# Pooled-query attention and a two-layer MLP on one core: transposes one tile late, large scores as split products, row sums spread through DRAM

## The reference

```
q_pool = q.reshape(B, H, S // 2, 2, D).mean(axis=3)          # B=4, H=8, S=1152, D=64
scores = (1 / sqrt(D)) * q_pool @ k.T                        # 576 x 1152 for each head
attn   = exp(scores - max(scores));  attn /= sum(attn) + 1e-09
x      = (attn @ v), heads side by side                      # 2304 tokens x 512
h      = x @ w_in                                            # w_in 512 x 2048
out    = (max(h, 0) + alpha * min(h, 0)) @ w_out             # w_out 2048 x 512
```

## Time and profile before

| | us |
|---|---|
| median of three runs | 931.33 (930.55 to 931.39) |
| profiled execution, its own time | 932.26 |
| its span | 929.7 |
| PE busy | 887.3 (95% of the span) |
| DVE busy | 516.9 (56%) |
| ACT busy | 423.4 (46%) |
| POOL busy | 213.3 (23%) |

### The profile page before, as it was taken

The page is one execution under the profiler, slowest core; times in us unless marked ns, Lnnn a source line. Parts: engine busy times, 40 slices in busy tenths (PEclk is TensorE's granted clock), DMA queues, the critical chain, the costliest instruction groups (busy, mean ns, idle before and its releaser), DMA issues. The chain is left out here.

```text
span 929.7 us, 20770 instructions
## 1 busy us (share of the span) xinstructions
PE 887.3 (95%) x6896; PEld 623.2 (67%) x6896; DVE 516.9 (56%) x836; ACT 423.4 (46%) x963; POOL 213.3 (23%) x182
## 2 busy tenths in 40 slices
PE   3799999999999999999999999999999999999997
PEld 1455555555555555555545799989999999989995
DVE  2676767677767776767676344344444444343442
ACT  2566666666666666666666222222322222322222
POOL 2112111211121112111200323323232323323230
PEclk9999999999999999999999999999999999999999
DMA  7435423542354235523520122212422222322211
GB/s 186 106 83 135 119 65 82 133 121 63 82 133 123 60 82 133 127 57 82 133 71 1 59 68 58 67 62 63 136 57 68 57 68 61 132 59 66 65 36 68
DMA packets 36366, 79.57 MB, mean 86 GB/s; under 512 B 5360, under 2 KB 9456, under 8 KB 36336
## 3 DMA queue, kind: packets, MB, share of 16 engines
q1 hardware_dynamic: 33936, 74.48, 31.0%
q10 hardware_dynamic: 2400, 4.72, 1.5%
HBM read 74.46 MB, written 4.72 MB: 85 GB/s over the span
## 5 line engine op out<-in xcount | busy, mean ns | idle before, releaser
L432 DVE TENSOR_REDUCE neg_max<-s_ps 128x1 f32<-128x1152 f32 x144 | 194.1, 1348 | 16.6 <-DVEq L431 16.6
L573 PE MATMUL pv_ps<-pt,v_f 128*64 128x256 f32 (+1 forms) x1152 | 169.0, 414 | 0.0
L532 PE MATMUL s_ps<-k_f,q_f 64*128 64x512 f32 (+1 forms) x640 | 160.2, 626 | 5.2 <-PEq L543 5.2
L348 ACT ACTIVATE e_sb<-s_ps,neg_max 128x1024 f32<-128x1024 f32 x144 | 160.1, 1112 | 0.0
L587 PEld LDWEIGHTS slot_ps<-ident,e_sb 64*128 64x128 f32 x2304 | 86.0, 139 | 82.4 <-issue 82.4
L465 DVE COPY pt<-slot_ps 128x512 f32<-128x512 f32 x144 | 99.6, 692 | 61.3 <-DVEq L464 59.4
L341 ACT ACTIVATE e_sb<-s_ps,neg_max 128x128 f32<-128x128 f32 x144 | 52.9, 367 | 171.5 <-ACTq L340 171.5
L617 PE MATMUL slot_ps<-x_hi,wi_hi 128*128 128x384 f32 x384 | 129.5, 337 | 1.1 <-PEq L613 1.1
L617 PE MATMUL slot_ps<-x_lo,wi_hi 128*128 128x384 f32 x384 | 129.5, 337 | 0.0
L617 PE MATMUL slot_ps<-x_hi,wi_lo 128*128 128x384 f32 x384 | 129.0, 336 | 0.0
L479 DVE TENSOR_SCALAR e_sb<-slot_ps,alpha_sb 128x384 f32<-128x384 f32 x96 | 59.3, 618 | 123.2 <-DVEq L477 123.2
(11 more groups left out here) (46 smaller groups left out, 1098.8 us busy)
## 6 DMA issues: line engine op xcount, KB each, us to landing
q_raw<-in_q SPq DMA_DIRECT2D x64, 288.0 KB, 4.5
k_f<-in_k SPq DMA_DIRECT2D x64, 288.0 KB, 4.2
wi_raw<-in_w_in SPq DMA_DIRECT2D x48, 256.0 KB, 2.6
wo_raw<-in_w_out SPq DMA_DIRECT2D x48, 256.0 KB, 2.6
v_f<-in_v SPq DMA_DIRECT2D x32, 288.0 KB, 3.0
out<-pt ACTq DMA_DIRECT2D x6, 768.0 KB, 4.4
k_end<-in_k SPq DMA_DIRECT2D x64, 32.0 KB, 4.0
alpha_sb<-in_alpha SPq DMA_DIRECT2D x1, 8.0 KB, 4.7
```

Of the source, the lines that this page charges most:

```text
L348: nc.scalar.activation(e_sb[:, b * NKEY + at:b * NKEY + at + n], s_ps[:, S_AT[b] + at:S_AT[b] + at + n], ACT.Exp, bias=neg_max[:, b:b + 1] ...
L432: nc.vector.tensor_reduce(out=neg_max[:, b:b + 1], in_=s_ps[:, S_AT[b]:S_AT[b] + NKEY], op=ALU.max, axis=AX_X, negate=True).then_inc(max_r ...
L532: ins = nc.tensor.matmul(s_ps[to:to + m, S_AT[b] + at:S_AT[b] + at + BANK], q_f[2 * g + h][rows, first:first + m], k_f[2 * g + h][rows, at ...
L573: ins = nc.tensor.matmul(pv_ps[h * D:(h + 1) * D, 0:n], v_f[2 * g + h][:, a, :], pt[:, a, at:at + n], start=(a == 0), stop=(a == KT - 1))
```

## The change

It has several parts.

- *Lagging transposes.* Step s now transposes tile s-1, not s, before the large scores of s+2. The wait for the exponential of tile s moves behind the transposes, `e_sb` holds three tiles, and there is one step more (`REST + 1`). The tables `PRODUCT`, `INVERT` and `SCALE` move by one step.
- *Ninth block through the second bank.* `NINTH` is now the first 128 columns of `slot_ps[1]`. PE waits (`half1_copied`) until DVE has copied that bank before it transposes the ninth block, and the bank comes free only when DVE has copied the ninth block too.
- *Split large scores.* q and k are each held as an fp32r high part and the rest, and a piece of 512 columns is the sum of three fp32r matmuls, taken in turn on the upper and lower row half. The mixed tile uses 128-column queries with zeros in the place of the other head (640 query columns in place of 576, `WIDE`), so it takes six matmuls for each piece. POOL makes the parts (for the first heads DVE and ACT do), POOL also cuts `k_end` from the loaded keys, and `k_raw` is a single staging buffer.
- *Sums through DRAM.* `spread_inverse` and the copy of its result are gone. SP stores the inverse sums to DRAM and reads them back onto 64 partitions each; the columns of the tiles are reordered so that they come out in a row.
- *x and its split.* `scale` writes float32 results to `x_f`. POOL splits those of the first pass before the MLP (`x_split`); in the last hidden block of each further pass ACT takes the high part (`x_high`) and DVE the rest (`x_low`), in the space that the split keys had.

The core of the diff:

```diff
-    NQ = q.shape[3]
+    NQ = NKEY // 2
+    QCOLS = q.shape[3]
...
-    SOURCE = [[(0, 0, P, 0)], [(1, 0, P, 0)], [(0, P, P, 0)], [(1, P, P, 0)],
-              [(0, 2 * P, HALF, 0), (1, 2 * P, HALF, HALF)],
-              [(0, 320, P, 0)], [(1, 320, P, 0)], [(0, 448, P, 0)], [(1, 448, P, 0)]]
-    PT_AT = [0, 320, 128, 448, 256, 640, 896, 768, 1024]
-    PT_MIX = 576
+    SOURCE = [[(0, 0, P, 0)], [(1, P, P, 0)], [(0, P, P, 0)], [(1, 2 * P, P, 0)],
+              [(0, 2 * P, HALF, 0), (1, HALF, HALF, HALF)],
+              [(0, 3 * P, P, 0)], [(1, 3 * P, P, 0)], [(0, 4 * P, P, 0)], [(1, 4 * P, P, 0)]]
+    WIDE = [[(h, col) for h, col, _, _ in tile] for tile in SOURCE]
+    WIDE[MIX] = [(0, 2 * P), (1, 0)]
+    assert QCOLS == NQ + HALF
...
-    PRODUCT = {5: (0, (0, 1)), 6: (0, (2, 3)), 7: (0, (4, 5)), 8: (0, (6, 7, 8)),
-               0: (1, (0, 1)), 1: (1, (2, 3)), 2: (1, (4, 5)), 3: (1, (6, 7)), 4: (1, (8,))}
-    SPREAD = {6: 0, 1: 1}
-    INVERT = {4: 0, 8: 1}
-    FIRST = 6
+    PRODUCT = {6: (0, (0, 1)), 7: (0, (2, 3)), 8: (0, (4, 5)), 0: (0, (6, 7, 8)),
+               1: (1, (0, 1)), 2: (1, (2, 3)), 3: (1, (4, 5)), 4: (1, (6, 7)), 5: (1, (8,))}
+    INVERT = {5: 0, 0: 1}
+    SCALE = {1: 0, 6: 1}
+    FIRST = 7
...
-        NINTH = s_ps[:, 2 * BANK + P:2 * BANK + 2 * P]
+        NINTH = slot_ps[1][:, 0:P]
...
+            def store_sums(group):
+                a, b = GROUP_TILES[group]
+                sp.wait_ge(inv_ready, 1).then_inc(inv_ready, -1)
+                sp.dma_start(sums[a * P:b * P].rearrange("(t p) -> p t", p=P), inv_sum[:, a:b],
+                             allow_slow_non_contiguous=True).then_inc(inv_stored, 16)
+            def spread_sums(group):
+                _, _, n, first = GROUPS[group]
+                sp.wait_ge(inv_stored, 16).then_inc(inv_stored, -16)
+                for h in range(2):
+                    row = sums[GROUPS[group][h]:GROUPS[group][h] + n]
+                    sp.dma_start(inv_bc[h * D:(h + 1) * D, first:first + n],
+                                 row.rearrange("(o n) -> o n", o=1).to_broadcast([D, n])).then_inc(inv_bc_in[group], 16)
...
+            with sp.Fori(0, NPAIR // 2 - 2) as two:
                 for g in range(2):
-                    load_pair(two * 2 + g, g)
+                    store_sums(0), spread_sums(0)
+                    load_q_raw(two * 4 + 7 + 2 * g)
+                    store_sums(1)
+                    load_k_raw(two * 4 + 7 + 2 * g)
+                    spread_sums(1)
+                    load_v_pair(two * 2 + 2 + g, g)
+                    load_qk(two * 4 + 8 + 2 * g)
...
+            def split_q(i, raw, done):
+                pool.wait_ge(done, 32).then_inc(done, -32)
+                nc.gpsimd.tensor_tensor(raw[:, 0, :], raw[:, 0, :], raw[:, 1, :], ALU.add).then_inc(pool_self, 1)
+                pool.wait_ge(pool_self, 1).then_inc(pool_self, -1)
+                nc.gpsimd.tensor_scalar(q_f[i][:, :], raw[:, 0, :], QSCALE, 1.0, ALU.mult,
                                         ALU.mult).then_inc(pool_self, 1)
                 pool.wait_ge(pool_self, 1).then_inc(pool_self, -1)
+                nc.gpsimd.tensor_copy(q_hi[i], q_f[i][:, :]).then_inc(pool_self, 1)
+                pool.wait_ge(pool_self, 1).then_inc(pool_self, -1)
+                nc.gpsimd.tensor_tensor(q_lo[i], q_f[i][:, :], q_hi[i].bitcast(F32),
+                                        ALU.subtract).then_inc(pool_self, 1)
+                pool.wait_ge(pool_self, 1).then_inc(pool_self, -1)
                 pool.sem_inc(q_ready[i], 1)
+            def split_qk(i):
+                split_q(i, q_raw, q_raw_in)
                 pool.sem_inc(q_raw_free, 1)
...
+                pool.wait_ge(k_raw_in, 32).then_inc(k_raw_in, -32)
+                nc.gpsimd.tensor_copy(k_hi[i], k_raw[:, :]).then_inc(pool_self, 1)
+                pool.wait_ge(pool_self, 1).then_inc(pool_self, -1)
+                nc.gpsimd.tensor_tensor(k_lo[i], k_raw[:, :], k_hi[i].bitcast(F32), ALU.subtract).then_inc(pool_self, 1)
+                pool.wait_ge(pool_self, 1).then_inc(pool_self, -1)
+                nc.gpsimd.tensor_copy(k_end[i][0:D, :, :], key_ends(k_raw[0:D, :])).then_inc(pool_self, 1)
+                pool.wait_ge(pool_self, 1).then_inc(pool_self, -1)
+                pool.sem_inc(k_ready[i], 1)
+                pool.sem_inc(k_raw_free, 1)
+            def split_pair(g):
+                pool.wait_ge(qk_free[g], 1).then_inc(qk_free[g], -1)
+                split_qk(2 * g), split_qk(2 * g + 1)
...
                 t, g = s % TILES, s // TILES % 2
                 if left > 0:
                     exponential_cut(s + 1)
-                act.wait_ge(tr_ready[0], 1).then_inc(tr_ready[0], -1)
-                nc.scalar.activation(pt_half(t, 0), half_columns(slot_ps[0][:, :]), ACT.Copy).then_inc(slot_free[0], 1)
+                if s > 0:
+                    act.wait_ge(tr_ready[0], 1).then_inc(tr_ready[0], -1)
+                    nc.scalar.activation(pt_half((s - 1) % TILES, 0), half_columns(slot_ps[0][:, :]),
+                                         ACT.Copy).then_inc(slot_free[0], 1)
                 if left > 0:
                     exponential(s + 1)
-                if t in SPREAD and (t == 6 or pair is not None):
...
-                if t == TILES - 2:
-                    act.sem_inc(k_free[g], 1)
-                    act.sem_inc(q_free[g], 1)
+                if t == TILES - 2 and left > 0:
+                    act.sem_inc(qk_free[g], 1)
...
+            def x_high(n, h):
+                nc.scalar.activation(x_part(x_hi, h), x_chunk(n, h), ACT.Copy).then_inc(x_hi_done, 1)
...
             def step(s, pair, left=2):
                 t, g = s % TILES, s // TILES % 2
-                if t == 0 and pair is not None:
-                    dve.wait_ge(x_sb_free, 1).then_inc(x_sb_free, -1)
-                    scale(0)
-                if t == 5 and pair is not None:
-                    scale(1)
-                    dve.sem_inc(v_free[1 - g], 1)
-                dve.wait_ge(tr_ready[1], 1).then_inc(tr_ready[1], -1)
-                nc.vector.tensor_copy(pt_half(t, 1), half_columns(slot_ps[1][:, :])).then_inc(slot_free[1], 1)
-                if t in INVERT:
+                if t in SCALE and pair is not None:
+                    scale(SCALE[t], pair + (0 if s < 2 * TILES else 1))
+                    if SCALE[t] == 1:
+                        dve.sem_inc(v_free[1 - g], 1)
+                if s > 0:
+                    dve.wait_ge(tr_ready[1], 1).then_inc(tr_ready[1], -1)
+                    nc.vector.tensor_copy(pt_half((s - 1) % TILES, 1),
+                                          half_columns(slot_ps[1][:, :])).then_inc(half1_copied, 1)
+                if t in INVERT and (INVERT[t] == 0 or pair is not None):
                     invert(INVERT[t])
-                if t == 5 and pair is not None:
-                    x_high(pair + (0 if s < 2 * TILES else 1))
-                dve.wait_ge(bank2_ready, 1).then_inc(bank2_ready, -1)
-                nc.vector.tensor_copy(pt_ninth(t), ninth_columns(t)).then_inc(ninth_free, 1)
+                if s > 0:
+                    dve.wait_ge(ninth_ready, 1).then_inc(ninth_ready, -1)
+                    nc.vector.tensor_copy(pt_ninth((s - 1) % TILES), NINTH).then_inc(slot_free[1], 1)
                 if left > 1:
+                    dve.wait_ge(bank2_ready, 1).then_inc(bank2_ready, -1)
                     row_max(s + 2)
...
+                def x_low(h):
+                    dve.wait_ge(x_hi_done, 1).then_inc(x_hi_done, -1)
+                    nc.vector.tensor_tensor(x_part(x_lo, h), x_chunk(n + 1, h), x_part(x_hi, h).bitcast(F32),
+                                            ALU.subtract).then_inc(x_ready, 1)
                 def hidden(f, i, first, last):
                     unit(f, 0)
                     if n == 0 and not first:
-                        scale(1)
-                        x_high(NPAIR - 1)
+                        scale(1, NPAIR - 1)
+                    if last and not last_pass:
+                        x_low(0)
                     unit(f, 1)
+                    if last and not last_pass:
+                        x_low(1)
...
             def big_scores(s):
-                t, b, g = s % TILES, s % 2, s // TILES % 2
-                pieces = []
-                for row, at in enumerate(BIG[b]):
-                    rows = slice(row * HALF, (row + 1) * HALF)
-                    for h, first, m, to in SOURCE[t]:
-                        ins = nc.tensor.matmul(s_ps[to:to + m, S_AT[b] + at:S_AT[b] + at + BANK],
-                                               q_f[2 * g + h][rows, first:first + m],
-                                               k_f[2 * g + h][rows, at:at + BANK], start=True, stop=True)
-                    pieces.append(ins)
+                b, g = s % 2, s // TILES % 2
+                terms = []
+                for h, col in WIDE[s % TILES]:
+                    i = 2 * g + h
```

(50 more changed lines are left out.)

307 lines of the change are left out of this document (165 added, 142 removed).

## The result

The changed kernel takes 1017.83 us (median; 1011.52 to 1023.79) against 931.12 before: ratio 1.093, 95% interval 1.0865 to 1.0998. The forecast was 944.2, its range 908 to 970. Slower was right; the size was not. The profiled execution is the fastest of the four, 1011.52 us, against 932.26 before.

The account below looks back on a forecast made before the run. The prediction took PE to bound the attention. From the profiled 932.26 us, pairs +8.7, start -2, end +3.5 less 0.6 and pass boundaries +3.2 gave 945.1, a median of 944.2 us, range 908 to 970.

Parts of the forecast that it names:

- spreads gone: Attention on PE: dropping the six small matmuls that spread sums, at t = 6 and t = 0, saves 1.36 us per pair.
- The wait for the half copy: Each attention step: the ninth block waits for DVE's copy of its bank and starts at T+1.72 us, before at 1.56.
- The pair: Nine attention steps for two heads, t = 6 to t = 5: 31.49 us against 30.91, or +8.7 over fifteen pairs.
- ripple through `scale` at t = 6: DVE at t = 6: `scale` delays the half copy from 0.88 to 1.97, making the step 4.52 us, not 3.43.
- the sums through DRAM "at nothing": Sum DMAs replacing the spreading cost nothing, as their result is wanted over 15 us later, against a load's few us.
- With SP's queue also blocked by the two sum stores: Rival: q and k reach PE late through SP, staging and POOL; +2.5 per pair, 982 us; chance 0.08 including blocked DVE.
- By the rule only `x_low` and the first `k_lo` could be hit: DVE and POOL sharing a port pair: POOL's new load could block only these DVE operations, which alters no pair.
- Start: First heads: extra q and k operations against earlier loading and lagging transposes; between -6 and +6 us, taken as -2.
- End: End of the attention: one more step without scores costs +3.5 us, less 0.6 for the last spreading.
- Pass boundaries: Two MLP pass boundaries: `x_low` on DVE and ACT's part cost nothing to 4.5 us each; taken as 1.6, together +3.2.
- fast rival: Rival: the ninth block is not held and starts at 1.40, -2.5 us per pair, 907 us; chance 0.24, whole or partly.
- Halves in turn: Rival: score matmuls of upper and lower row half wait for each other, +4.0 us per pair, 1008 us; chance 0.11.

Follow-up runs that it names:

- e5: Changed kernel with e1's reduction and e2's store together, rows scaled by other rows' sums: 959.86 us, ratio 1.0298 to the kernel before.
- e7: e5 with the ninth block back in the small scores' bank, rows scaled by other rows' sums: 910.55 us, ratio 0.9771.
- e6: Changed kernel with e1's reduction, ninth block in the small scores' bank, and sums spread by PE matmuls and an ACT copy, not through DRAM: 930.76 us, ratio 0.9988.
- e10: e5 with only the product of the high parts, one term of three, in the large scores: 972.22 us, ratio 1.0442.
- e8: Changed kernel with e1's reduction, ninth block in the small scores' bank, and sum stores and spreading issued by ACT instead of SP: 989.10 us, ratio 1.0633.
- e1: Changed kernel with the two-input addition of row sums on DVE made a reduction with one SBUF input, 1e-9 dropped: 984.08 us, ratio 1.0566.
- e2: Changed kernel with inverse sums stored as 128 descriptors, not 640 (512) single elements, so rows get other rows' sums: 982.64 us, ratio 1.0531.
- e9: Changed kernel with e1's reduction, ninth block in the small scores' bank, and sums turned by a matmul, then stored as 512-byte rows: 921.00 us, ratio 0.9888.
- e11: e9 with x_low made by a copy instead of the subtraction, so x's low part is wrong from the second pass: 918.03 us, ratio 0.9854.

## Why the prediction was wrong

*Bound, spreads gone, exponential's wait gone.* PE as the bound was right of before and of the clean pair (e5, e7), not of the changed kernel. The six matmuls' 1.36 was near: e6 and e7 differ by 1.26 a pair.

*The wait for the half copy.* Right, place and size: T+1.72 forecast, T+1.73 measured; e7 gives T+1.40 for the rival, as forecast; e10 shows that the length of the scores does not matter. Scores 0.88: right (0.88 in e7), side by side.

*The pair.* The terms of the forecast add up to 31.47 (31.49 was a slip). Against e5, from t = 6: 4.52 forecast, 4.58 measured; 3.43, 3.50; 3.43, 3.50; 3.97, 4.04; 3.41, 3.6 to 3.7; 3.58, 3.58; 3.21, 3.28; 3.21, 3.3; 2.71, 2.86. In all 0.85 too little per pair, and 11.7 us over the fifteen, as the first takes only 31.50. Of the 0.85, ninth block to product, kept at 0.48 and really 0.54, is 0.06 in each of eight steps. The rest is mostly t = 1, where the half copy behind `scale` comes at up to T+1.32, not T+1.09, and t = 5, where the product takes 0.58 and not 0.51. The ripple through `scale` at t = 6 was right.

*The failed step: the sums through DRAM "at nothing".* I set "a load's few us" against the 15 us until the result is wanted. The rows of loads carried whole rows; a store of single elements stood in no row of before and should have been bounded by its number of packets. It took 7.7 to 12.0 us, and through SP it pushed the loads and its own return past `scale`. "With SP's queue also blocked by the two sum stores" stood in a rival, priced at 2.5 a pair with a chance of 0.08; e8 shows that a free queue of SP alone would not have saved it, since loads land late beside such stores on another queue too. Alone it was 24 us (e1 to e5), 35 beside the lock (e2).

*The second failed step: "By the rule only `x_low` and the first `k_lo` could be hit".* By the earlier trace rows the half copies could not be hurt, and they were not (680 to 693 ns after). But `invert` adds two SBUF inputs as well, and I overlooked it. The Trainium skill, "SBUF — State Buffer", section "SBUF: two separate sides", says that of a DVE operation with two SBUF inputs and a GpSimd operation that reads SBUF, the one that starts first takes the shared port pair for its whole instruction, and the other waits. The trace agrees: POOL's subtraction had begun 0.48 us earlier, and the addition took 2.17 us for 0.155 and ended with it. Alone this was 23 us (e2 to e5, the clock's falls in e2 included), 34 beside the store (e1).

*POOL at nothing* was right as a bound: 44 to 62% busy from 100 to 300 us in all runs with it. *Start*, by e5: the transposes of the first t = 6 are 0.4 ahead of before, for a forecast of 2. *End*, by e5: from the transposes of the last t = 6 to the first MLP matmul it is 14.9 us, before 10.6: +4.3 for a forecast of +2.9. *Pass boundaries*: +3.2 forecast; e9 and e11 give 3.2, by `x_low`, and the MLP of e5 takes 3.4 more than before.

So the forecast's 945.1 for a profiled execution becomes e5's 960.2 by the pair (11.7), the start (1.6), the end (1.4) and 0.2 in the MLP; the changed kernel's 1017.8 comes by the store and the lock. The forecast's fast rival, 907, was right of e7: 910.6. "Halves in turn", 1008, came near the result by accident; the halves do run together.

*Open.* PE stood 5.65 us at 108 to 114 us with nothing that the profile shows as its cause ("issue"), beside a sum store; e1 has a like step (7.38), e2 and e5 do not. The trace has one packet of 16 KB of an instruction queue there, from 111.22 to 112.39, and e1 has one from 110.39 to 111.62; PE goes on 1.45 us after its end in both. So a wait for program code is likely, but no run tests it. Nor is the share of the lower clock in the 58 us settled: it was at 0.50 from 76.5 to 90.1 and from 110.6 to 117.4 us, but only after PE had stopped, and three short falls after 160 us cost about 1.5 us each if they cost what they do in e2.
